# A reordered attention-only stage in a fused attention and double-MLP kernel

## The reference

```python
state = np.zeros((B, H, D, D))                 # B, H, S, D = 4, 8, 768, 48
for t in range(S):
    cur = np.einsum('bhd,bhe->bhde', u[None] * kt, vt)
    y[:, :, t] = np.einsum('bhd,bhde->bhe', rt, state + cur)
    state = w[None, :, :, None] * state + np.einsum('bhd,bhe->bhde', kt, vt)
x = y as (3072, 384)
h = x @ w_in;  x = (np.maximum(h, 0) + alpha * np.minimum(h, 0)) @ w_out    # 384 -> 2048 -> 384
h = x @ w_in2; out = (h * np.tanh(softplus(h))) @ w_out2                    # 384 -> 2048 -> 384
```

## Time and profile before

| | us |
|---|---|
| median of 3 runs (1006.86 to 1009.42) | 1007.99 |
| the profiled execution, its own time | 1006.3 |
| its span, first to last instruction | 1004.4 |
| PE busy | 961.3 |
| DVE busy | 674.5 |
| ACT busy | 622.1 |
| POOL busy | 374.6 |
| start of the first MLP's first `up` | 79.58 |

### The profile page before, as it was taken

One profiled execution on the slowest core, in us unless ns is written; L12 is line 12 of the kernel. 1 busy time (PEld: TensorE's weight loads), 2 busy tenths in 40 slices (PEclk: granted clock), 3 DMA queues, 4 the chain that ended last, 5 costly groups with the idle time before them and its releaser, 6 DMA issues.

```text
span 1004.4 us, 23889 instructions
## 1 busy us (share of the span) xinstructions
PE 961.3 (96%) x9476; PEld 792.4 (79%) x9476; DVE 674.5 (67%) x1370; ACT 622.1 (62%) x1268; POOL 374.6 (37%) x663
## 2 busy tenths in 40 slices
PE   4678999999999999999999999999999999999998
PEld 3666777888888888888887888888888888888886
DVE  7668777666666666656663345877767777777775
ACT  5545555554555555455544667877777777787775
POOL 8768776667666667666610440000000000000000
PEclk9958999999999999999999999999999999999999
DMA  6223442212121122211103232000000000000000
GB/s 182 54 81 93 127 117 73 77 49 58 45 76 45 46 77 55 61 46 61 30 5 146 79 96 94 32 0 32 32 32 23 10 31 0 0 31 0 32 1 31
DMA packets 24610, 54.29 MB, mean 54 GB/s; under 512 B 4928, under 2 KB 12736, under 8 KB 24512
## 3 DMA queue, kind: packets, MB, share of 16 engines
q1 hardware_dynamic: 22640, 43.43, 14.9%
q10 hardware_dynamic: 1872, 9.49, 2.3%
HBM read 41.10 MB, written 9.44 MB: 50 GB/s over the span
## 4 chain that ended last, share of the span: by engine, by line
PE 93%; DVE 3%; issue 2%; ACT 1%; DMA 0%; SPq 0%; ACTq 0%; DVEq 0%
PE acc L990 39%; PE hid L974 29%; PE lev L974 10%; PE lev L1032 8%; PE tok L1055 2%; PE tok L1049 2%; PE tok L1006 1%; DVE scores L584 1%; PE hid L1032 1%; PE acc L1049 0%; DMA x_parts<-y 0%; PE acc L1055 0%; SPq L313 0%; DVE w_lo L670 0%; DVE arena L302 0%
## 5 line engine op out<-in xcount | busy, mean ns | idle before, releaser
L974 PE MATMUL hid<-x_parts,w_hi 128*128 128x512 f32 x864 | 291.2, 391 | 7.7 <-DMA x_parts<-y 5.4
L990 PE MATMUL acc<-g_hi,w_hi 128*128 128x512 f32 x576 | 230.8, 401 | 0.0
L990 PE MATMUL acc<-g_hi,w_lo 128*128 128x512 f32 x576 | 224.9, 390 | 0.0
L974 PEld LDWEIGHTS hid<-x_parts,w_hi 128*128 128x128 f32 x864 | 163.0, 189 | 43.4 <-issue 8.9
L584 DVE COPY_PREDICATED scores<-mask,lev 64x128 f32<-64x128 int8 x430 | 153.3, 357 | 46.1 <-ACT scores L831 24.0
L974 PE MATMUL hid<-x_parts,w_lo 128*128 128x512 f32 x432 | 168.9, 391 | 0.0
L867 ACT ACTIVATE relu_neg<-hid 128x512 f32<-128x512 f32 x96 | 57.4, 598 | 170.9 <-PE hid L974 170.9
L990 PE MATMUL acc<-g_lo,w_hi 128*128 128x512 f32 x576 | 162.2, 390 | 0.0
L676 DVE SCALAR_TENSOR_TENSOR hid<-relu_neg,neg_slope,hid 128x512 f32<-128x512 f32 x96 | 72.5, 755 | 113.5 <-ACT hid L868 113.3
L990 PEld LDWEIGHTS acc<-g_hi,w_hi 128*128 128x128 f32 x576 | 108.0, 187 | 23.7 <-issue 0.2
L990 PEld LDWEIGHTS acc<-g_lo,w_hi 128*128 128x128 f32 x576 | 108.1, 188 | 23.0
(11 more groups left out here) (88 smaller groups left out, 1343.3 us busy)
## 6 DMA issues: line engine op xcount, KB each, us to landing
w_raw<-weights SPq DMA_DIRECT2D x32, 384.0 KB, 3.1
arena<-rkv SPq DMA_DIRECT2D x24, 384.0 KB, 3.4
arena<-rk_t SPq DMA_DIRECT2D x48, 192.0 KB, 3.6
arena<-rkv SPq DMA_DIRECT2D x24, 192.0 KB, 2.6
x_dram<-result ACTq DMA_DIRECT2D x6, 768.0 KB, 3.6
arena<-x_dram SPq DMA_DIRECT2D x6, 768.0 KB, 4.3
out<-result ACTq DMA_DIRECT2D x6, 768.0 KB, 3.3
x_parts<-y SPq DMA_DIRECT2D x141, 16.0 KB, 1.8
```

What stands on the lines that cost most here:

```text
L974: last = nc.tensor.matmul(to[:, 0:TILE], w[:, j, kt * P:(kt + 1) * P], x[:, par, kt], start=x is x_hi and w is w_hi and kt == 0, stop=x is ...
L990: last = nc.tensor.matmul(acc[d][:, 0:TILE], w[:, j, cols], g[:, j % RING], start=j == 0 and g is g_hi and w is w_hi, stop=j == STEPS - 1 ...
```

## The change

`FIRST` becomes 10. Scores and state get three buffers, `y3` two, and the holes two semaphores by parity. On SP the loads of a chunk go ahead of the holes of chunk c - 3. On DVE `advance_state` goes ahead of the picks, the key levels go behind them, and the first two splits of weights move. On ACT the fills of the diagonal move. On POOL `rows_for_state(c - 1, x = 1)` moves behind the next chunk's first queries. Banks change place so that unit 9 can be scored beside the MLP.

```diff
-FIRST = CHUNKS_PER_TILE * PER_CHUNK + 1
+FIRST = (CHUNKS_PER_TILE + 1) * PER_CHUNK
+HELD = 3
-        scores = sb("scores", [P, 2, 2, 2, CHUNK])
-        state = sb("state", [P, 2, PAIRS, D])
-        y3 = sb("y3", [P, 2, CHUNK], F32R)
+        scores = sb("scores", [P, HELD, 2, 2, CHUNK])
+        state = sb("state", [P, HELD, PAIRS, D])
+        y3 = sb("y3", [P, 2, 2, CHUNK], F32R)
...
-            c = (s + 17) // 4
-            return c if s % 4 == 3 and c < CHUNKS else None
+            c = (s + 19) // 4
+            return c if s % 4 == 1 and c < CHUNKS else None
...
+            if rep == 0 and v == FIRST - 1:
+                return acc_all[:, 1:3]
+            return hid_pair if rep == 0 and v % PER_CHUNK else lev
...
-            engine.wait_ge(xlo_done, c + 1)
             for q in halves:
+                engine.wait_ge(ylo_done if q else xlo_done, c + 1)
@@ sync @@
-            for c in range(2, CHUNKS_PER_TILE + 1):
+            for c in range(2, CHUNKS_PER_TILE + 2):
+                load_rows(c)
                 load_rk(c + 1)
-                load_rows(c)
+                if c > 2:
+                    fill_holes(sp, c - 3)
                 load_v(c)
-                fill_holes(sp, c - 2)
+                if c == 3:
+                    load_weights(3)
+            fill_holes(sp, CHUNKS_PER_TILE - 1, (0,))
+            for i in (4, 5):
+                load_weights(i)
@@ gpsimd, first_tile @@
                 queries_of(0, 0, 1)
+                scale_for_state(0, 0, 1)
                 products(1, 1, 1)
...
                     queries_of(c, par, 0)
+                    if c > 1:
+                        rows_for_state(c - 1, 1 - par, 1)
                     scale_for_state(c, par, uses)
                     queries_of(c, par, 1)
                     rows_for_state(c, par, 0)
                     products(c + 1, 1 - par, (c + 1) // 2 + 1)
-                    rows_for_state(c, par, 1)
+                rows_for_state(CHUNKS_PER_TILE, CHUNKS_PER_TILE % 2, 1)
@@ vector, advance_state @@
-                reached(dve, av_done, PER_CHUNK * c)
+                reached(dve, av_done, PER_CHUNK * (c - 1))
@@ vector, first_tile @@
-                    if l == 1:
-                        power_by_token()
+                power_by_token()
...
+                split_lo(0)
                 dve.wait_ge(s_masks, 2 * LOW + 2)
                 for v in range(FIRST):
                     c, x = divmod(v, PER_CHUNK)
+                    ends, between = c == CHUNKS_PER_TILE, None
+                    if x == 0:
+                        advance_state(c, token_bank(0, c))
+                    if ends and x == 0:
+                        between = lambda n: x_lo_part(c - 1, 0, c - 1, token_bank(0, c - 1)) if n == LOW - 1 else None
+                    pick_scores(v, 0, between)
+                    if not ends:
                         level = scale_half(c + 1, x, False)
-                        between = lambda n: level(n - 1) if 1 < n <= LEVELS else None
+                        for l in range(1, LEVELS):
+                            level(l)
                     if x == 0:
-                        if 0 < c < CHUNKS_PER_TILE:
+                        if 0 < c and not ends:
                             x_lo_part(c - 1, 0, c - 1, token_bank(0, c - 1))
-                        advance_state(c, token_bank(0, c))
                         sum_diagonal(c + 1, (c + 1) % 2)
-                for i in range(1, LAG1 + 1):
-                    split_lo(i)
+                split_lo(1)
@@ vector, tile1 @@
                     lo_part(s, j)
+                    if t == 1 and j < STEPS - EARLY and j + EARLY not in pool_slots:
+                        split_lo(j + EARLY)
                     if unit is not None:
                         pick_scores(unit, 1)
...
-                    if t == 1 and 0 < j < STEPS - EARLY and j + EARLY not in pool_slots:
-                        split_lo(j + EARLY)
@@ scalar, first_tile @@
-                slot_before = {1: 0, 3: 1, 5: 2}
+                slot_before = {0: 0, 3: 1, 5: 2}
...
-                    fill_diagonal(v)
+                    if x == 0:
+                        fill_diagonal(v)
                     if v in slot_before:
                         split_hi(slot_before[v])
                     copy_high(v, 0)
-                    if x == 0 and c > 0:
-                        x_hi_part(c - 1, 0, c - 1, token_bank(0, c - 1))
+                    if x == 0:
+                        fill_diagonal(v + 1)
+                        if c > 0:
+                            x_hi_part(c - 1, 0, c - 1, token_bank(0, c - 1))
+                        if c == CHUNKS_PER_TILE:
+                            fill_holes(act, c - 1, (1,))
                 fill_diagonal(FIRST)
-                fill_holes(act, CHUNKS_PER_TILE - 1, (1,))
```

More of the change, by code:

```diff
@@ L147, in build @@
         hid = [hid_pair[:, i] for i in range(2)]
-        acc = [bank(f"acc{i}") for i in range(KT)]
+        acc_all = ctx.enter_context(nc.psum_tensor("acc", [P, KT, 512], F32))
+        acc = [acc_all[:, i] for i in range(KT)]
         lev = ctx.enter_context(nc.psum_tensor("lev", [P, 2, 512], F32))
@@ L151, in build @@
         hid2 = hid + [lev[:, i] for i in range(2)]
-        rev_table = acc[0][:, 0:PAIRS * HALF].rearrange("p (a t) -> p a t", a=PAIRS)
-        fwd_table = acc[2][:, 0:PAIRS * HALF].rearrange("p (a t) -> p a t", a=PAIRS)
+        rev_table, fwd_table = (acc[1][:, i * PAIRS * HALF:(i + 1) * PAIRS * HALF].rearrange("p (a t) -> p a t", a=PAIRS)
+                                for i in range(2))
         x2_dram = nc.dram_tensor("x2_dram", (TILES, P, KT, TILE), F32, kind="Internal").ap()
@@ L192, in build @@
         av_done = sem("av_done")
-        holes_in = sem("holes_in")
+        holes_in = [sem(f"holes_in{i}") for i in range(2)]
+        ylo_done = sem("ylo_done")
         xhi_done = sem("xhi_done")
@@ L312, in fill_holes @@
                     holes = x_parts[HALF * q + D:HALF * (q + 1), odd, :, k, cc * CHUNK:(cc + 1) * CHUNK]
-                    engine.dma_start(holes.bitcast(F32), y3[first:first + HALF - D].bitcast(F32)
-                                     ).then_inc(holes_in, 16)
+                    engine.dma_start(holes.bitcast(F32), y3[first:first + HALF - D, c % 2].bitcast(F32)
+                                     ).then_inc(holes_in[c % 2], 16)
         @block.sync
@@ L549, in power_by_token @@
                 dve.wait_ge(s_ptr, 1)
-                nc.vector.tensor_copy(power_tok[:], acc[1][:].rearrange(
+                nc.vector.tensor_copy(power_tok[:], acc[0].rearrange(
                     "p (a h d) -> p a h d", a=PAIRS, h=2)[:, :, :, 0:D]).then_inc(s_ptok, 1)
             def advance_state(c, bank):
-                now, new = state[0:ROWS, c % 2], state[0:ROWS, 1 - c % 2]
-                reached(dve, av_done, PER_CHUNK * c)
+                now, new = state[0:ROWS, c % HELD], state[0:ROWS, (c + 1) % HELD]
+                reached(dve, av_done, PER_CHUNK * (c - 1))
                 if ends_sequence(c):
@@ L817, in fill_diagonal @@
                         h = 2 * (2 * x + u) + q
-                        last = nc.scalar.activation(scores[:, x, q, u], ident[:], ACT.Copy, scale=diag[:, c % 2, h:h + 1])
+                        last = nc.scalar.activation(scores[:, v % HELD, q, u], ident[:], ACT.Copy, scale=diag[:, c % 2, h:h + 1])
                 last.then_inc(fill_done, 1)
             def copy_high(v, rep):
-                x = v % PER_CHUNK
                 act.wait_ge(score_done, v + 1)
@@ L827, in copy_high @@
                     m = 1 << l
-                    src = level_scores(level_banks(rep, x), l)
+                    src = level_scores(level_banks(rep, v), l)
                     rows, tokens = slice(2 * m * b, 2 * m * b + m), slice(2 * m * b + m, 2 * m * (b + 1))
                     first = m * b if l == LEVELS - 1 else m * b % QUARTER
-                    nc.scalar.activation(scores[rows, x, :, :, tokens].rearrange("p q u n -> p (q u) n"),
+                    nc.scalar.activation(scores[rows, v % HELD, :, :, tokens].rearrange("p q u n -> p (q u) n"),
                                          src[rows, :, first:first + m], ACT.Copy).then_inc(high_picked, 1)
@@ L873, in tile1 @@
                     hi_part(s, j)
+                    if coming is not None:
+                        fill_diagonal(coming)
                     if unit is not None:
@@ L955, in _ @@
             for p in range(PAIRS):
-                last = nc.tensor.transpose(acc[1][:, p * P:(p + 1) * P], power_rev[:, p], ident[:])
+                last = nc.tensor.transpose(acc[0][:, p * P:(p + 1) * P], power_rev[:, p], ident[:])
             last.then_inc(s_ptr, 1)
@@ L965, in up @@
                 if holes is not None:
-                    pe.wait_ge(holes_in, holes)
+                    for i in range(2):
+                        pe.wait_ge(holes_in[i], holes)
                 if split is not None:
@@ L1048, in attend @@
```

(4 more changed lines are left out.)

42 lines of the change are left out of this document (15 added, 27 removed).

## The result

The changed kernel takes 998.76 us (median of 4 runs, 995.74 to 999.02) where the kernel before takes 1007.99. The ratio is 0.9901, 95% interval 0.9878 to 0.9924. That is 9 us faster, where 18.4 were forecast: about half, and just outside the range, whose upper end was 998. The profiled execution has a span of 997.2 us against 1004.4, 7.2 less.

A forecast was written before the change was run, and what follows sets the result against it. PE, busy 961.3 of 1004.4 us, bounds the kernel; its first stage is bound by waits. 13.0 + 2.6 + 2.8 = 18.4 off 1007.99 gives 989.6, stated as 989.5; forecast 984 to 994 (0.66), range 984 to 998.

The forecast's parts named there:

- The first stage: Chunks before the MLP: with loads ahead of holes, 11.0 us a chunk on DVE; first `up` at 66.6 instead of 79.58, 13.0 us.
- The unit moved ahead: Unit 9 scored before the MLP: one score and one `attend` leave the part where PE is the bound, 2.6 us.
- The first MLP steps: First `up` to `up` of step 4: `w_lo` stall goes, 20.7 us where 23.53 stood, 2.8 us gained.
- My 20.7 us: Forecast time from first `up` to `up` of step 4, with `up` 0 at full clock.
- the terms I listed: PE's own work 17.6; waits of `attend(9)` 1.2, `up` 2 0.4 and `attend(10)` 1.2 us.
- The first `up` at half clock: Start of the MLP: full clock was assumed for `up` 0; half clock would cost 2.1 us more.
- rival 4: First MLP steps: DVE becomes the bound for 12 more steps and `up` 0 is at half clock; 8 us back, 998; chance 0.07.
- Rival 2: DVE waits for POOL's instructions at `advance_state` and splits; 4 to 6 us back, about 995; 0.22 together with rival 1.
- Rivals 1 and 3: 1: first-stage engines couple, 996, 0.22 with rival 2. 3: weights late, `up` 4 to 15 stall, 1016, 0.04.
- One sign that I had listed as wrong: POOL idle on a DMA, listed among the signs that the prediction is wrong; no size given.

The follow-up runs named there:

- the fourth experiment: Changed kernel with the splits of weights in the MLP's steps put back behind the picks, as before: 997.23 us, ratio 0.9908.
- the trace pair: Best version with nine units before the MLP, against best version with `split_lo(1)` ahead of unit 9's picks: spans 989.1 and 985.9 us.
- the last four versions: State ahead of `lo_part` (992.61 us); the best version (988.80); on it, `split_lo(1)` ahead of unit 9's picks (988.03) or nine units before the MLP (991.85).
- the best version: Changed kernel plus `advance_state(5)` early, later `advance_state` ahead of `lo_part`, and POOL waiting for its own completions: 988.80 us, ratio 0.9816.

## Why the prediction was wrong

- **"The first stage", 13.0: right in mechanism, 10.8 measured.** DVE's cycle of 11.0 us a chunk came about as worked out, except in chunk 3: even scores start at 22.67, 32.99, 43.65 and 56.10. `advance_state` of chunks 1 to 4 began at 27.3, 38.2, 49.0 and 61.3, forecast 26.6, 37.6, 48.6, 59.6. Of the 1.7 at the end 0.7 are from the start (`split_lo(0)` took 1.83 beside POOL), and the rest is mostly one state step of 2.13 us; in the fourth experiment, with the same first stage, that step took 0.48 and the first `up` came at 66.61, the 66.6 of the forecast. Another half microsecond is in the last holes, 4.1 from `x_lo_part` to `up` instead of 3.5. The experiments weigh the parts: taking back DVE's order costs more than taking back SP's. The forecast had told the stage by SP's holes first.
- **"The unit moved ahead", 2.6: right in size.** 3.2 by the trace pair, 3.8 by the medians, and 3.8 in the stretch after `up` 4.
- **"The first MLP steps", 2.8: the step that failed; it was -7.4.** I followed the waits of `attend(10)` for DVE's picks and stopped there. `attend` waits for four things (the values, the state, the scaled rows, the scores), and `state_done` for its chunk is one. Before the change the same wait stood in steps 3 and 4, hidden behind the `up` that waited for `w_lo` until 103.11: by the time PE came, at 105.41, the state was 0.1 us old. The change takes that cover away and moves the state to step 1, where DVE is 3.8 us late from the long split. My 20.7 us for these steps was not wrong as a sum of work, though the terms I listed (17.6, 1.2, 0.4 and 1.2) add up to 20.4: with the wait and the long split taken out it is 21.2, and 20.4 with the split in DVE's idle time. The 10.2 us between 20.7 and 30.9 are, by the rows: 3.4 more wait before `attend(10)`, 3.9 of half clock behind it, 2.9 of half clock in the first `up` and `attend(9)`, 0.9 on `w_lo`, less 1.2 that `attend(9)` didn't wait; 0.3 is left.
- **The first `up` at half clock.** I took full clock since PE would have few gaps. The windows of 56 to 68.8 us show a granted clock of 0.50 after gaps of up to 2.3 us in 44 to 56. It was named, with its 2.1, as the alternative. Only this half of rival 4 occurred; that its 998 is what was measured is chance.
- **Rival 2** (DVE waits for POOL's instructions) was priced at 4 to 6 us by the largest row then seen, 1.1 for a split. It is real, and the price was of another kind: not one instruction of POOL but many in a row, 3.8 us for one split. The Trainium skill, SBUF — State Buffer (section "SBUF: two separate sides"), has the lock for one instruction; the 3.57, 4.75 and 7.46 us here span 6, 9 and 14 of POOL's, so the measurement goes further than its sentence.
- **Rivals 1 and 3, and the steps of rival 4,** didn't occur. The chunks took 10.3 to 12.5; PE had no stall over 0.8 us after `up` 4; the later steps gained. One sign that I had listed as wrong did show: POOL idled 7.1 us for a DMA of `rk_t`, until 86.12, behind the weights in SP's queue. PE never waited for it.

Open: how much of the 2.13 us state step is due to which of POOL's instructions, and why a DVE instruction gets in at some changes between POOL's and not at others. It is not that it is long: a later split in the kernel after got in among six levels without a pause, and so did `split_lo(1)` at 78.86 in the run with DVE's order of before, in 1.00 us. DVE and POOL, after:

```profile
89.91 1.71 DVE L681 TENSOR_TENSOR w_lo<-w_raw,w_hi 128x768 fp32r<-128x768 f32 x1
```

```profile
88.81 3.13 POOL L297 TENSOR_TENSOR arena<-arena,power 112x128 f32<-112x128 f32 x6
```

## What to carry to other kernels

When a stall is taken away, list every semaphore that the released instruction waits for, with the time at which each is signalled in the old trace, and look at the one just under the old stall: it is next. Then ask whether the instruction needs what it waits for. An update that only a later stage reads (here a memset, 0.22 us) belongs where its inputs are ready, not at the end of the list. Moving the memset alone showed nothing in the whole time, since the same wait stood one chunk on; moving the later updates too, ahead of `lo_part`, in a gap that DVE had anyway, was worth 0.5%. And a stall on PE is to be priced with the half clock behind it, which here nearly doubled it.

## What the runs showed of the hardware

- A DVE `tensor_tensor` with both inputs in SBUF can be kept out by many back-to-back GpSimd instructions. The split of 0.95 us took 3.57, 4.75 and 7.46 us behind 6, 9 and 14 of them, 5.28 with satisfied semaphore waits between them, and 1.19 when GpSimd waited for its own completion behind each. The price of these waits was 0.6 us per six instructions. It is no rule for every such run of instructions: other splits got in beside six of them in 1.71 and 1.00 us.
- PE idle for 4.56 us had a granted clock of 0.55 over the 8.67 us that followed, and idle for 3.28 us one of 0.75 over 13.8 us. Short gaps went both ways: ahead of `attend(12)` PE idled for 1.02, 0.97, 1.02 and 0.97 us in the last four versions. The clock fell soon after in two of them (0.66 over 4.5 us with the state ahead of `lo_part`, 0.72 over 6 us in the best version) and stayed at 1.00 in the other two. Such a dip costs about 1.5 us, an estimate from these windows; what decides on it, and whether the gap is its cause, is not shown.
